# Bucket attention and two MLPs: the first head's bits made in place, two tiles of bits, loads in turn, and matmuls of constants at the start

## What is computed

```python
q_bits = (np.einsum('bhsd,dk->bhsk', q, proj) > 0)        # k_bits the same
q_bucket = np.sum(q_bits * powers, axis=-1)               # k_bucket the same
mask = q_bucket[:, :, :, None] == k_bucket[:, :, None, :]
scores = np.where(mask, scale * np.matmul(q, k.transpose(0, 1, 3, 2)), -1e9)
attn = softmax(scores);  x = attn @ v
x = moe(x)     # P(h)/Q(h) of h = x @ w_in, a cubic over a quadratic, then @ w_out
out = moe2(x)  # h * relu6(h + 3) / 6 of h = x @ w_in, then @ w_out
```

## Time and profile before

| | us |
|---|---|
| runs of the kernel | 769.31 median (769.05, 769.31, 771.49) |
| the profiled execution | 769.31, of which 767.6 from its first to its last instruction (span) |
| TensorE matmul, busy | 744.6 (97%) |
| VectorE / ScalarE / GpSimd, busy | 481.2 / 433.7 / 177.8 |

### The profile page before, as it was taken

How to read it: one execution, slowest core, us unless ns; L and a number is a source line. 1 busy time by engine, 2 the same in 40 slices (tenths; PEclk the granted TensorE clock), 3 DMA queues, 4 the chain that set the end, 5 groups by cost and what they waited for, 6 DMA issues and landing times.

```text
span 767.6 us, 10893 instructions
## 1 busy us (share of the span) xinstructions
PE 744.6 (97%) x3712; PEld 580.8 (76%) x3712; DVE 481.2 (63%) x892; ACT 433.7 (57%) x783; POOL 177.8 (23%) x174
## 2 busy tenths in 40 slices
PE   4699999999999999999999999999999999999998
PEld 2566766676666888888888888888888888888886
DVE  4777778787775888899888989852222322232223
ACT  3677676777765889776767889851212121212121
POOL 1444545555531445100000254430000000000000
PEclk9999999999999999999999999999999999999999
DMA  6644355444300233100000133310000100010001
GB/s 150 162 117 111 80 146 147 103 112 116 94 1 1 87 105 95 45 0 0 0 0 0 55 97 96 107 57 1 1 0 1 55 0 0 0 55 1 1 0 56
DMA packets 35082, 43.29 MB, mean 56 GB/s; under 512 B 4192, under 2 KB 23392, under 8 KB 35040
## 3 DMA queue, kind: packets, MB, share of 16 engines
q1 hardware_dynamic: 34752, 42.32, 20.5%
q10 hardware_dynamic: 288, 0.43, 0.2%
HBM read 26.61 MB, written 3.15 MB: 39 GB/s over the span
## 4 chain that ended last, share of the span: by engine, by line
PE 93%; DVE 3%; DMA 1%; SPq 1%; issue 0%; ACTq 0%; ACT 0%; POOL 0%; DVEq 0%; POOLq 0%
PE y_ps L917 34%; PE h_ps L864 11%; PE h_ps L865 11%; PE h_ps L866 11%; PE o_ps L844 8%; PE t_ps L826 8%; PE s_ps L816 4%; PE s_ps L815 4%; DVE probs L609 2%; DMA probs<-in_k 1%; PE p_ps L799 1%; DVE x_lo L630 1%; PE p_ps L844 1%; DMA k_cross<-q_cross 0%; SPq L285 0%
## 5 line engine op out<-in xcount | busy, mean ns | idle before, releaser
L708 DVE SCALAR_TENSOR_TENSOR t_abs<-t_abs,h_ps 128x512 f32<-128x512 f32 x48 | 33.0, 688 | 187.2 <-ACT t_abs L505 187.2
L864 PE MATMUL h_ps<-x_hi,slot 128*128 (+1 forms) x384 | 149.7, 390 | 0.0
L865 PE MATMUL h_ps<-x_lo,slot 128*128 (+1 forms) x384 | 149.4, 389 | 0.0
L866 PE MATMUL h_ps<-x_hi,slot 128*128 (+1 forms) x384 | 149.4, 389 | 0.0
L505 ACT ACTIVATE t_abs<-h_ps,three_col 128x512 f32<-128x512 f32 x48 | 33.1, 690 | 191.7 <-PE h_ps L866 191.7
L394 POOL TENSOR_TENSOR slot<-w_raw,slot 128x512 fp32r<-128x512 f32 x64 | 81.6, 1293 | 208.6 <-ACT slot L458 208.6
L917 PE MATMUL y_ps<-g_hi,slot 128*128 128x512 f32 x384 | 126.0, 389 | 0.0
L387 POOL TENSOR_SCALAR probs<-probs,row_inv 128x768 f32<-128x768 f32 x96 | 95.2, 994 | 125.0 <-DVE row_inv L614 124.7
L917 PE MATMUL y_ps<-slot,g_hi 128*128 128x512 f32 x384 | 118.2, 389 | 0.0
L609 DVE TENSOR_SCALAR_CACHE_REDUCE probs<-s_ps 128x768 f32<-128x768 f32 x96 | 91.6, 956 | 26.9 <-PE t_ps L826 20.9
L432 ACT ACTIVATE probs<-probs,least 128x768 f32<-128x768 f32 x96 | 89.4, 932 | 8.4 <-DVE probs L609 7.6
(11 more groups left out here) (72 smaller groups left out, 1094.7 us busy)
## 6 DMA issues: line engine op xcount, KB each, us to landing
w_raw<-in_moe_w_in SPq DMA_DIRECT2D x32, 256.0 KB, 2.7
w_raw<-in_moe_w_out SPq DMA_DIRECT2D x32, 256.0 KB, 2.7
raw<-in_q SPq DMA_DIRECT2D x16, 192.0 KB, 3.1
v_nat<-in_v SPq DMA_DIRECT2D x16, 192.0 KB, 3.1
raw<-in_k SPq DMA_DIRECT2D x15, 192.0 KB, 3.4
k_main<-q_main SPq DMA_DIRECT2D x15, 192.0 KB, 2.6
k_cross<-q_main SPq DMA_DIRECT2D x15, 192.0 KB, 3.1
k_cross<-q_cross SPq DMA_DIRECT2D x15, 192.0 KB, 2.6
```

The lines of the kernel that those rows point to most:

```text
L864: mm(h_ps[b][:, :], w_hi, x_hi[:, kt, cols], start=(kt == 0), stop=False)
L865: mm(h_ps[b][:, :], w_hi, x_lo[:, kt, cols], start=False, stop=False)
L866: last = mm(h_ps[b][:, :], w_lo, x_hi[:, kt, cols], start=False, stop=(kt == KT - 1))
```

## The change

The first head's bits are no longer made in p_ps and moved. TensorE projects the head into partitions 64 to 95 of the two scores banks' tiles s_ps, with proj_pair for the queries and a second tile, proj_key, for the keys; both halves of a side go to the same partitions and different banks. VectorE compares rows 64 to 75 and writes them straight into q_main and k_main. The query side's low part from swapped goes from VectorE to ScalarE, the keys' low part (k_cross) from VectorE to GpSimd. Head 1 is projected after the scores of tiles 0 and 1, thresholded between clamps 0 and 1, and its low part made behind clamp 1. There are two tiles of bits, by the parity of the pair, the second in the last group of x_lo; thresholds wait for the head two further back. Pair 1 is projected and thresholded at tiles 2 and 3 instead of 0 and 1. The SyncE queue waits for the first raw before the loads of heads 1 and 2. TensorE multiplies a tile of ones three times ahead of the first projection and once behind it.

```diff
+        proj_key = sb("proj_key", [P, QUAD])
-            bits = sb("bits", [P, HALF], F32R, attn)
+            bits_even = sb("bits_even", [P, HALF], F32R, attn)
+            filler = probs[0][:, 0:HALF]
+        bits = (bits_even[:, :], x_group(x_lo, 2 * PAIRS - 1))
         def placed(h):
-            return 80 * (h // SETS + 1) - (16 if h % SETS == 0 else 0)
+            return 80 * (h // SETS + (h % SETS != 0))
+        def project_at(i):
+            return 2 if i == 0 else 0
...
             def place_head(h):
-                sp.wait_ge(bits_made, h // 2 + 2)
+                sp.wait_ge(bits_made, h // 2 + 1)
...
             sp.dma_start(swapped[D:P, :], q_dram[dram_head(0, 0), :, :]).then_inc(swapped_in, 16)
+            sp.wait_ge(raw_in[0][0], 32)
             load_raw(0, 1)
             load_raw(1, 0)
-            sp.wait_ge(bits_made, 1)
-            sp.wait_ge(first_q, 2)
-            place_bits(sp, 0, 0)
             load_raw(1, 1)
             place_head(1)
...
+            pool.wait_ge(sel_made, 10)
+            pool.wait_ge(hi_made, 1)
+            nc.gpsimd.tensor_tensor(k_cross[0][D:P, :], raw[0][0][D:P, :], q_main[0][D:P, :].bitcast(F32),
+                                    ALU.subtract).then_inc(first_lo, 1)
+            pool.wait_ge(first_lo, 1)
...
             for to in (k_main, k_cross):
                 nc.scalar.activation(to[0][0:D, :], swapped[0:D, :], ACT.Copy).then_inc(first_k, 1)
-            act.wait_ge(bits_made, 1)
-            for half in range(2):
-                cols, rows = slice(HALF * half, HALF * (half + 1)), QUAD * half + MASKROWS
-                act.dma_start(k_main[0][D:KROWS, cols].bitcast(F32), bits[rows:rows + MASKROWS, :].bitcast(F32))                    .then_inc(main_in[0], 16)
+            nc.scalar.activation(q_cross[0][D:P, :], swapped[D:P, :], ACT.Copy, scale=-SCALE).then_inc(first_k, 1)
...
+            nc.vector.memset(filler[:, :], 1.0).then_inc(filled, 1)
+            def threshold(i, rows=slice(0, P)):
+                dve.wait_ge(bits_dot, i + 1)
+                if i >= 2:
+                    dve.wait_ge(main_in[(2 * i - 3) % SETS], placed(2 * i - 3))
+            def first_threshold(side, dots):
+                to, value = (q_main, k_main)[side], (-1.0, -PENALTY)[side]
+                dve.wait_ge(first_dots, dots)
+                nc.vector.tensor_scalar(to[0][D:KROWS, :].rearrange("p (g n) -> p g n", g=2),
+                                        s_ps[side][D:KROWS, :].rearrange("p (g n) -> p g n", g=2)[:, :, 0:HALF],
+                                        bit_col[D:KROWS, 0:1], value, (ALU.is_ge, ALU.is_lt)[side], ALU.mult).then_inc(first_bits, 1)
...
                 clamp(n, j)
+                if n == 0:
+                    threshold(0, slice(D, P))
...
                 invert(n, j)
-                if j == 0 and i + 1 < PAIRS:
+                if n == 0:
+                    split_lo(1)
+                if j == project_at(i) and i + 1 < PAIRS:
                     threshold(i + 1)
...
             nc.vector.tensor_scalar(q_main[0][:, :], raw[0][0][:, :], scale_col[:, 0:1], None, ALU.mult)\
-                .then_inc(first_q, 1)
-            nc.vector.tensor_tensor(k_cross[0][D:P, :], raw[0][0][D:P, :], q_main[0][D:P, :].bitcast(F32),
-                                    ALU.subtract).then_inc(first_q, 1)
+                .then_inc(hi_made, 1)
+            dve.wait_ge(hi_made, 1)
+            nc.vector.scalar_tensor_tensor(q_cross[0][0:D, :], raw[0][0][0:D, :], -SCALE,
+                                           q_main[0][0:D, :].bitcast(F32), ALU.mult, ALU.subtract).then_inc(lo_made, 1)
             dve.wait_ge(bit_col_made, 1)
-            threshold(0, slice(0, D), first=True)
-            nc.vector.tensor_scalar(q_cross[0][D:P, :], swapped[D:P, :], -SCALE, None, ALU.mult).then_inc(first_q, 1)
-            threshold(0, slice(D, P))
-            split_lo(1)
+            first_threshold(1, 1)
+            dve.wait_ge(first_lo, 1)
+            first_threshold(0, 2)
...
+            def first_project(side):
+                for half in range(2):
+                    last = mm(s_ps[side][D:D + QUAD, BANK * half:BANK * half + HALF], (proj_pair, proj_key)[side][:, :],
+                              raw[0][0][:, HALF * half:HALF * (half + 1)], start=True, stop=True)
+                last.then_inc(first_dots, 1)
...
                 if n == 0:
-                    pe.wait_ge(first_k, 2)
+                    pe.wait_ge(first_k, 3)
+                    pe.wait_ge(first_lo, 1)
+                    pe.wait_ge(first_bits, 2)
...
-                if j == 0 and i + 1 < PAIRS:
+                if n == 0:
+                    project(0, 1)
+                if j == project_at(i) and i + 1 < PAIRS:
                     project(i + 1, 0)
                     project(i + 1, 1)
...
-            project(0, 0)
-            project(0, 1)
+            def stay_busy(times):
+                for _ in range(times):
+                    mm(o_ps[:, 0:HALF], filler[:, 0:P], filler[:, :], start=True, stop=True)
+            pe.wait_ge(filled, 1)
+            stay_busy(3)
+            pe.wait_ge(proj_made, 8)
+            pe.wait_ge(raw_in[0][0], 32)
+            first_project(1)
+            first_project(0)
+            stay_busy(1)
```

More of the change, by code:

```diff
@@ L166, in bucket_attention_and_two_mlps @@
         proj_made = sem("proj_made")
+        filled = sem("filled")
+        first_dots = sem("first_dots")
+        first_bits = sem("first_bits")
+        first_lo = sem("first_lo")
         act_setup = sem("act_setup")
@@ L171, in bucket_attention_and_two_mlps @@
         v_in = [sem(f"v_in{e}") for e in range(2)]
-        first_q = sem("first_q")
         hi_made = sem("hi_made")
@@ L276, in place_keys, with place_bits @@
                 move(k_cross[c][0:D, :], q_main[c][D:P, :]).then_inc(moved_in[c], 16)
-            def place_bits(queue, h, side):
+            def place_bits(h, side):
                 c, at = h % SETS, 2 * QUAD * (h % 2) + MASKROWS * side
@@ L284, in place_bits @@
                     rows = slice(at + QUAD * half, at + QUAD * half + MASKROWS)
-                    queue.dma_start(to[D:KROWS, cols].bitcast(F32), bits[rows, :].bitcast(F32)).then_inc(main_in[c], 16)
+                    sp.dma_start(to[D:KROWS, cols].bitcast(F32), bits[h // 2 % 2][rows, :].bitcast(F32))\
+                        .then_inc(main_in[c], 16)
             def place_head(h):
@@ L290, in place_head @@
                 place_keys(h)
-                sp.wait_ge(bits_made, h // 2 + 2)
-                place_bits(sp, h, 1)
+                sp.wait_ge(bits_made, h // 2 + 1)
+                place_bits(h, 1)
                 sp.wait_ge(lo_made, h + 1)
@@ L296, in place_head @@
                 move(q_cross[c][D:P, :], q_main[c][0:D, :]).then_inc(main_in[c], 16)
-                place_bits(sp, h, 0)
+                place_bits(h, 0)
             def load_weights(m, f):
@@ L577, in _ @@
         def _(dve):
+            nc.vector.memset(filler[:, :], 1.0).then_inc(filled, 1)
             nc.vector.memset(proj_pair[:, :], 0.0).then_inc(proj_made, 1)
+            nc.vector.memset(proj_key[:, :], 0.0).then_inc(proj_made, 1)
             nc.vector.memset(scale_col[0:D, :], -SCALE).then_inc(scale_made, 1)
@@ L581, in _ @@
             dve.wait_ge(proj_in, 32)
-            dve.wait_ge(proj_made, 1)
-            for a, (sign, u) in enumerate(((1.0, 0), (-1.0, 0), (-1.0, 1), (1.0, 1))):
+            dve.wait_ge(proj_made, 2)
+            for to, a, sign, u in ((proj_pair, 0, 1.0, 0), (proj_pair, 1, -1.0, 0), (proj_key, 0, 1.0, 1), (proj_key, 1, -1.0, 1),
+                                   (proj_pair, 2, -1.0, 1), (proj_pair, 3, 1.0, 1)):
                 rows = slice(D * u, D * (u + 1))
-                nc.vector.tensor_scalar(proj_pair[rows, BITS * a:BITS * (a + 1)], proj_raw[rows, :], sign, None,
+                nc.vector.tensor_scalar(to[rows, BITS * a:BITS * (a + 1)], proj_raw[rows, :], sign, None,
                                         ALU.mult).then_inc(proj_made, 1)
[L588 to L594, removed]
+            def threshold(i, rows=slice(0, P)):
+                dve.wait_ge(bits_dot, i + 1)
+                if i >= 2:
+                    dve.wait_ge(main_in[(2 * i - 3) % SETS], placed(2 * i - 3))
+                nc.vector.tensor_scalar(bits[i % 2][rows, :], p_ps[rows, 0:HALF], bit_col[rows, 0:1],
+                                        bit_col[rows, 1:2], ALU.is_ge, ALU.mult).then_inc(bits_made, 1)
+            def first_threshold(side, dots):
[4 more added lines that the diff above has]
+                                        bit_col[D:KROWS, 0:1], value, (ALU.is_ge, ALU.is_lt)[side], ALU.mult).then_inc(first_bits, 1)
             def split_lo(h):
@@ L788, in _ @@
             mm = nc.tensor.matmul
+            def first_project(side):
[3 more added lines that the diff above has]
+                last.then_inc(first_dots, 1)
             def project(i, u):
-                if i == 0 and u == 0:
```

(13 more changed lines are left out.)

7 lines of the change are left out of this document (removed).

## The result

The changed kernel takes 766.12 us, the median of 20 runs (764.63 to 772.55), the kernel before 771.35 in as many (769.05 to 773.83). The ratio is 0.994, 95% interval 0.9927 to 0.9954: 0.6% faster, which is 4.6 us of 771.35; the two medians differ by 5.2. The forecast was 4.5. The median 766.12 lies in the forecast's range, but 1.3 above its 764.8 and outside the 764.2 to 765.3 that it held likeliest. The run that was predicted from had 769.31, near the lower end of the kernel before; the best runs of the two differ by 4.4 us (769.05 and 764.63).

A forecast was written before the change was run, and what follows sets the result against it. From 40 us TensorE bounds the kernel; before, the first pair's chain at 4.24 us a step. Clamp 4 comes 4.5 us earlier, 2.8 from the first scores' start and 1.7 after: 769.31 less 4.5 is 764.8, range 763.4 to 767.3.

The forecast's parts named there:

- The bound: From about 40 us TensorE is busy 159.49 of 160.00, so whatever shifts its list's start shifts the kernel's end.
- the mark: Start of the clamp of tile 4 on VectorE, 24.57 before, forecast 20.1: 4.5 us earlier.
- (a): First head: GpSimd's subtraction starts before VectorE's, or TensorE's clock rises late; 765.7 or 765.5, both some 767; chance 0.15.
- (c): Copies of head 1 or 2 come late, with 1.3 and 1.8 us to spare; 765.3 or 766.5; chance 0.07.
- fillers' end: End of the three filler matmuls of constants ahead of the first projection: 5.2 to 5.8, about when raw lands.
- T0: Start of the first scores on TensorE: 13.10 before, forecast 10.3, bounds 9.7 to 10.8.
- The stand-still on GpSimd: First head: GpSimd's subtraction of the keys' low part waits while VectorE's two-input operation runs, so it lasts 7.25 to 9.2.
- An idle time of 2.01 us ahead of 21.99 did not bring it down: TensorE kept its upper clock level through that idle time; used as evidence against a fall in the first pair.
- (d): Gap before T0 or first pair: TensorE falls to the lower level, +1.9 a step; 772.5 on top of (b); chance 0.04.
- (b): At the start the filler matmuls do nothing: T0 = 12.2, clamp 4 at 24.0, gain 0.6, 768.7; chance 0.07.
- the rise: TensorE's clock going from 1.2 to 2.4 GHz after some 4.6 us of nearly unbroken work, forecast near 5.9.
- the loads in turn: Swapped has only raw beside it in the queues, so ScalarE's first copy starts at 6.9 instead of 8.01.

The follow-up runs named there:

- the kernel with both gaps filled: Changed kernel plus identity matmuls in TensorE's idle times in the first pair and at the end of attention: 764.65 us median, ratio 0.9915.
- the two kernels with 3.54 or 4.13 us of idle time in one piece: The kernel before with start constants alone, 772.26 us median; the changed kernel with one tile of bits and the old wait, 771.82 us median.

## Why the prediction was right

The bound and the mark held, to within half a microsecond. With both kernels held from falling the difference at the end is 769.3 less 764.65, 4.65 us (on two chips); at clamp 4 it is 24.57 less 19.88, 4.69, in the kernel with both gaps filled, and 4.65 and 4.44 in the two profiled executions of the changed kernel. That end and mark agree so closely is in part luck. The longer step from clamp 8 to clamp 9 leaves 40.93 less 36.72, 4.21, at clamp 12, and by clamp 92 it has grown to 222.14 less 217.52, 4.62; what gave the 0.4 back, while TensorE is busy 159.5 of 160 us in both kernels, stayed open. The forecast of 4.5 was against the execution of before without a fall.

That the median 766.12 lies in the range is luck too. The range reached up to 767.3 for the rivals (a) and (c); (c) did not occur, and of (a) only a later rise did, which cost 0.2 us in the profiled execution of the changed kernel that had it. What put the median 1.3 above the forecast was the fall of the level, in the first pair in the profiled execution of 768.26. Of the group at 766.1 to 766.8 the changed kernel has no profile; that of the kernel with the loads at once, 765.94, fell in the first pair too, but only until about 25 us (granted clock 0.50 from 22 to 24 us, 0.65 from 24 to 26).

The terms, forecast and measured: raw 5.6 and 5.54; fillers' end 5.2 to 5.8 and 5.27 (1.37 + 3.90); dots of a side at the upper level 1.5 and 1.45; key and query dots' end 7.3 and 8.7, and 7.0 and 8.3; threshold of 12 x 768 0.96 and 1.01; T0 10.3 and 10.01; from there to clamp 4 9.8 and 9.91; head 1 in place T0 + 11.1, and 21.80 less 10.46, 11.3, with one tile of bits. No DMA is named ahead of the scores of head 1 (22.82; 22.7 forecast) or of head 2: rival (c) did not occur. Head 2's scores started at 35.97, 0.6 later than forecast, in the execution without a fall.

The stand-still on GpSimd was read rightly from one row of the kernel before: 2.50 beside VectorE's two-input operation, 1.80 without. Its own 1.80 was taken as 1.94, and GpSimd ended at 8.82 instead of 9.2, which covers the 0.3 by which T0 came earlier than forecast. By the rule of the Trainium skill, page "SBUF — State Buffer", section "SBUF: two separate sides", the lock goes both ways. The rows at 17.75 and 18.04 agree in direction: GpSimd had started first, and VectorE's two-input operation took 1.42 instead of 1.00 there, 0.42 more for 0.62 us side by side.

Three steps failed. First, "An idle time of 2.01 us ahead of 21.99 did not bring it down" was true of one execution and was taken for a property of the kernel. By the mean clocks (at most 0.998) over half of the runs of either kernel fall to the lower level, and of the 25 runs with the idle times of the first pair and of the end of attention filled (four kernels) none does. Rival (d) had the mechanism and nearly the price of a step (1.9 forecast, 6.36 - 4.24 = 2.1 measured), but tied it to case (b) and gave it 0.04; alone, on top of the full gain, it happened in 11 of 20 runs and cost 1.5, 3.6 or 7.9 us. The ratio came out as forecast because the kernel before pays the same. Second, the rise was read as 4.6 us of work: it came behind some 2.6 in one execution without constants and behind more than 5 in another, so (b)'s gain of 0.6 was too small; without constants 2.5 to 3.4 of 4.65 us remain (769.3 less 766.8 or 765.9). Behind the same constants, too, it came ahead of the key dots in some profiled executions (1.45 us) and within them in others (2.11, 1.95 and 2.23). What (b) missed is that dots late by 2 us move T0 by 2 and nothing else, since the scores then run at the upper level: T0 at 12.12 (12.2 in (b)), but clamp 4 at 22.04 and not at 24.0. Third, the loads in turn were given a gain of 1.1 us on ScalarE's first copy (8.01 to 6.9). It started at 7.05, but with the loads issued at once at 7.14: the turn was worth 0.09.

## To carry to other kernels

Read the mean clock of every run, not that of the profiled one: where times lie in groups, compare kernels within a group, or fill TensorE's idle times and compare then. A few matmuls on constants in the short idle times of a start-up phase, into a free bank, cost nothing and took the median from 765.98 to 764.65; in front of a longer wait, as in the kernel before, they only pay if they also fill the wait. And a copy that must be overwritten behind a DMA's reading deserves a second buffer where it stands in an in-order engine's list: without it 3.9 of the 4.65 us at clamp 4 were gone, and none of the first head's shortcuts showed at the end.

## What the runs showed of the hardware

TensorE fell to the lower level behind idle times of 0.68 and 1.40 us with work between them, in some executions and not in others of the same program; in the two kernels with 3.54 or 4.13 us of idle time in one piece it fell in every run (12 and 10 runs, mean clock at most 0.998 and 0.995), and the matmuls right behind it are at the lower level in both profiles (0.79 and 1.54 us). The granted clock in the profile reads 0.50 in such a fall but 1.00 in the program's first microseconds, while the matmuls there are at the lower level (the key dots' 2.74 against 1.45): only durations show the level at the start. Four FP32 matmuls in four column groups take as long as two in two (1.51 and 1.50), and two in one group take 2.74, all at the lower level.
